# Attention, a dense MLP and a soft mixture of experts on one core: two units opened side by side, a tail with halved copies and staggered loads

## What is computed

```python
for c in range(768 // 32):                    # chunked attention, 4 batches x 8 heads, head size 64
    k_full = concat(mem_k, k[16 before : 32 + 8 after])      # 8 memory keys + up to 56 keys
    a = softmax(q_c @ k_full.T / 8);  out[c] = a @ v_full
x = out as (3072, 512)
h = x @ w_in                                  # 512 x 2048
y = (h * sigmoid(h)) @ w_out                  # 2048 x 512
logits = y @ phi                              # 32 slots
slot_in = softmax(logits over tokens).T @ y   # (32, 512)
slot_out[e] = relu(slot_in[e] @ w1[e]) @ w2[e]       # 8 experts, 4 slots each, 512x1024 and 1024x512
result = softmax(logits over slots) @ slot_out
```

## Time and profile before

| | |
|---|---|
| three runs | 460.40, 461.74, 462.73 us (median 461.74) |
| the profiled execution | 461.4 us |
| its span, first to last instruction | 459.4 us |
| PE busy, share of the span | 442.7 us, 96% |
| PEld / DVE / ACT / POOL busy | 72% / 59% / 30% / 10% |
| mean granted PE clock | 0.994 of full |
| DMA | 81.57 MB, mean 178 GB/s |

### The profile page before, as it was taken

How to read it: one execution, slowest core, us unless ns; L and a number is a source line. 1 busy time by engine, 2 the same in 40 slices (tenths; PEclk the granted TensorE clock), 3 DMA queues, 4 the chain that set the end, 5 groups by cost and what they waited for, 6 DMA issues and landing times.

```text
span 459.4 us, 12251 instructions
## 1 busy us (share of the span) xinstructions
PE 442.7 (96%) x5438; PEld 330.8 (72%) x5438; DVE 272.7 (59%) x528; ACT 138.7 (30%) x257; POOL 47.4 (10%) x44
## 2 busy tenths in 40 slices
PE   6899999999999999999999999999999999999982
PEld 5798877778876778768787777887678779543551
DVE  5677746948477656487584785655664548541133
ACT  2666343232431423223234314233122222210022
POOL 2775100101001001010010010010000000010000
PEclk9999999999999999999999999999999999999997
DMA  8998244023050050230321402226200589999988
GB/s 303 412 414 337 99 156 173 1 93 116 2 201 9 17 191 1 93 118 0 111 97 60 150 1 86 100 93 277 92 0 0 208 358 419 340 418 424 420 357 356
DMA packets 14819, 81.57 MB, mean 178 GB/s; under 512 B 1584, under 2 KB 1712, under 8 KB 8880
## 3 DMA queue, kind: packets, MB, share of 16 engines
q1 hardware_dynamic: 14768, 80.81, 45.5%
HBM read 74.51 MB, written 6.29 MB: 176 GB/s over the span
## 4 chain that ended last, share of the span: by engine, by line
PE 89%; DMA 8%; DVE 1%; issue 0%; ACT 0%; DVEq 0%
PE h_ps L327 59%; DMA unit<-w 5%; PE lpu_ps L344 4%; PE sx_ps L284 4%; PE lpu_ps L375 4%; PE o_ps L311 3%; DMA qk_sb<-qk 3%; PE pt_ps L297 2%; PE sx_ps L375 2%; PE pt_ps L311 2%; PE h_ps L1081 2%; PE o_ps L1061 1%; PE lpu_ps L385 1%; PE sx_ps L1018 1%; PE h_ps L1018 1%; PE o_ps L344 1%
## 5 line engine op out<-in xcount | busy, mean ns | idle before, releaser
L327 PE MATMUL h_ps<-x_odd,w_pair 128*128 128x512 f32 x576 | 137.6, 395 | 0.0
L601 DVE SCALAR_TENSOR_TENSOR gT<-gT,h_ps 128x512 f32<-128x512 f32 (+1 forms) x112 | 67.8, 605 | 108.4 <-ACT gT L462 108.0
L327 PEld LDWEIGHTS h_ps<-x_odd,w_pair 128*128 128x128 f32 x576 | 106.4, 188 | 29.4 <-issue 5.9
L462 ACT ACTIVATE gT<-h_ps 128x512 f32<-128x512 f32 (+1 forms) x112 | 60.1, 536 | 214.2 <-PE h_ps L327 211.8
L327 PE MATMUL h_ps<-x_even,w_pair 128*128 128x512 f32 x384 | 92.4, 395 | 0.0
L327 PEld LDWEIGHTS h_ps<-x_even,w_pair 128*128 128x128 f32 x384 | 70.7, 188 | 19.6 <-issue 5.0
L609 DVE STREAM_TRANSPOSE gB<-gT 128x512 f32<-128x512 f32 x80 | 54.1, 696 | 0.8
L327 PE MATMUL h_ps<-x_short,w_pair 128*128 128x256 f32 x384 | 50.8, 287 | 0.4 <-DVE x_short L591 0.3
L585 POOL TENSOR_TENSOR sc<-sc,row_stats 128x512 f32<-128x512 f32 (+1 forms) x24 | 24.9, 1036 | 254.0 <-DVE row_stats L579 254.0
L327 PEld LDWEIGHTS h_ps<-x_short,w_pair 128*128 128x128 f32 x384 | 47.3, 191 | 4.6 <-issue 2.3
L472 ACT COPY pt<-pt_ps 64x512 f32<-64x512 f32 x46 | 26.5, 577 | 0.8
(11 more groups left out here) (183 smaller groups left out, 401.4 us busy)
## 6 DMA issues: line engine op xcount, KB each, us to landing
unit<-w SPq DMA_DIRECT2D x29, 1024.0 KB, 9.1
qk_sb<-qk SPq DMA_DIRECT2D x24, 640.0 KB, 5.9
v_sb<-v SPq DMA_DIRECT2D x24, 512.0 KB, 4.8
out<-unit SPq DMA_DIRECT2D x6, 1024.0 KB, 5.7
w_stage<-w_in SPq DMA_DIRECT2D x4, 1024.0 KB, 10.7
unit<-w_outT SPq DMA_DIRECT2D x4, 1024.0 KB, 13.5
unit<-w_out SPq DMA_DIRECT2D x4, 1024.0 KB, 6.0
unit_gT<-w SPq DMA_DIRECT2D x2, 1024.0 KB, 13.7
```

The source lines that it names most:

```text
L327: last = nc.tensor.matmul(h_ps[k % 2][:, 0:TOKS[b]], w_pair[:, k // 2, w, kc, k % 2 * 128:k % 2 * 128 + 128], x[:, lo, kc, 0:TOKS[b]], sta ...
L462: nc.scalar.activation(gt_of(b, k), h_ps[k % 2][:, 0:TOKS[b]], ACT.Tanh, scale=0.5).then_inc(tanh_done, 1)
L601: nc.vector.scalar_tensor_tensor(out=gt_of(b, k), in0=gt_of(b, k), scalar=1.0, in1=h_ps[k % 2][:, 0:TOKS[b]], op0=ALU.add, op1=ALU.mult).t ...
```

## The change

It touches the first 30 us and the last 60. In the first block's opening, unit 1 follows unit 0 step by step instead of one step behind: scores, sums, transposes and values of both come side by side, with own PSUM banks for unit 1 (`tr_of`, `o_of`). DVE normalises units 1 and 2 entirely, POOL all others. w_in(0) is issued ahead of v(0). Low parts 0 and 1 are computed in two halves with a semaphore count each, and low part 0 waits for DVE's normalise(1). Scores(3) and values(2) stand behind chunk 3 instead of chunk 2, and w_hi(2) and w_hi(3) come before tanh of chunks 1 and 2. In the tail, u is folded and copied in two halves of 256 columns (ACT and DVE), the slot inputs are turned and summed by one matmul with the fold matrix, five keep_busy calls are shorter or gone, the loads of the last ten tiles also wait for the tile three before, and the stores begin one tile earlier.

```diff
+STAGGERED = 10
-W_NEXT = {1: 3, 4: 4, 5: 5, 8: 6, 9: 7}
+W_NEXT = {1: 2, 2: 3, 4: 4, 5: 5, 8: 6, 9: 7}
-FIRST_SCORES = {2: 3, 6: 4, 10: 5, 11: 6, 13: 7}
-FIRST_VALUES = {2: 2, 6: 3, 10: 4, 13: 5}
+FIRST_SCORES = {3: 3, 6: 4, 10: 5, 11: 6, 13: 7}
+FIRST_VALUES = {3: 2, 6: 3, 10: 4, 13: 5}
...
         def pe_probs_T(pe, u):
-            pe.wait_ge(p_done, u + 1)
-            if u == 1:
-                pe.wait_ge(p_half, 1)
-            if u:
-                pe.wait_ge(pt_done, 2 * u)
+            if u in (1, 2):
+                pe.wait_ge(p_dve, u)
+            else:
+                pe.wait_ge(p_done, u - 1 if u else 1)
+            if u >= 2:
+                pe.wait_ge(pt_done, halves(u))
+                pe.wait_ge(pt_second, 2)
...
-            if b == 0 and q % 2 == 0:
-                pe.wait_ge(wl_done, 2 * n + q // 2 + 1)
+            if b == 0 and (k < 4 or q % 2 == 0):
+                pe.wait_ge(wl_done, k + 1 if k < 4 else k // 2 + 3)
...
         def low_part(ops, eng, m, done):
             eng.wait_ge(wh_done, m + 1)
-            ops.tensor_tensor(w_pair[:, m, 1, :, :], stage[:, m, 1, :, :], w_pair[:, m, 0, :, :].bitcast(fp32),
-                              ALU.subtract).then_inc(done, 1)
+            if m == 0:
+                eng.wait_ge(p_dve, 1)
+            for cols in (slice(0, 128), slice(128, 256)) if m < 2 else (slice(0, 256),):
+                ops.tensor_tensor(w_pair[:, m, 1, :, cols], stage[:, m, 1, :, cols], w_pair[:, m, 0, :, cols].bitcast(fp32),
+                                  ALU.subtract).then_inc(done, 1)
...
                 dve_g(dve, 0, k)
+                if k == 0:
+                    dve_sums(dve, 2)
+                    normalise(nc.vector, dve, 2, p_dve)
...
             load_qk(1)
-            load_v(0)
             sp.wait_ge(qk_in[0], 16)
             load_w_in(0)
+            load_v(0)
...
                 sp.wait_ge(s, count)
+                if u >= NU - STAGGERED:
+                    sp.wait_ge(unit_in[u - 3], 16)
                 sp.dma_start(units[where][:], sources[u]).then_inc(unit_in[u], 16)
...
-            sp.wait_ge(unit_in[NU - 2], 16)
+            sp.wait_ge(unit_in[NU - 3], 16)
...
-                normalise(nc.gpsimd, pool, n, 0, 4 if n == 1 else 2 * PAIRS, p_done)
+                if n not in (1, 2):
+                    normalise(nc.gpsimd, pool, n, p_done)
...
             act_exp(act, 1)
+            act_wh(act, 0)
             act_pt(act, 0)
-            act_wh(act, 0)
+            act_pt(act, 1)
             act_x(act, 0)
+            act_x(act, 1)
             act_wh(act, 1)
-            act_pt(act, 1)
-            act_x(act, 1)
             act_exp(act, 2)
-            act_wh(act, 2)
...
             dve_first_scores(dve)
+            dve_scores(dve, 1)
             dve_sums(dve, 0)
-            dve_scores(dve, 1)
-            pt_half(dve, nc.vector.tensor_copy, 0, 1)
             dve_sums(dve, 1)
-            normalise(nc.vector, dve, 1, 4, 2 * PAIRS, p_half)
+            normalise(nc.vector, dve, 1, p_dve)
+            pt_half(dve, nc.vector.tensor_copy, 0, 1, pt_second)
+            pt_half(dve, nc.vector.tensor_copy, 1, 1, pt_second)
             dve_x(dve, 0)
-            pt_half(dve, nc.vector.tensor_copy, 1, 1)
+            dve_x(dve, 1)
             dve_scores(dve, 2)
-            dve_x(dve, 1)
-            dve_sums(dve, 2)
...
             pe_scores(pe, 0)
-            keep_busy(2, h_ps[0])
             pe_scores(pe, 1)
             keep_busy(8, h_ps[0])
             pe_probs_T(pe, 0)
-            keep_busy(4, h_ps[0])
+            pe_probs_T(pe, 1)
             pe_values(pe, 0)
-            pe_probs_T(pe, 1)
+            pe_values(pe, 1)
             pe_scores(pe, 2)
-            pe_values(pe, 1)
-            keep_busy(4, h_ps[0])
+            keep_busy(1, h_ps[0])
...
-            nc.scalar.copy(uf[:], pt_ps[:]).then_inc(uf_cp, 1)
+            nc.scalar.copy(uf[:, 0:256], uf_ps[0][:, 0:256]).then_inc(uf_act, 1)
             act.wait_ge(uT_tr, 1)
-            nc.scalar.copy(uT, s_ps[:]).then_inc(uT_done, 1)
+            nc.scalar.copy(uT[:, 0:256], uT_ps[0][:, 0:256]).then_inc(uT_act, 1)
...
             for kc in range(KC):
-                last = nc.tensor.transpose(s_ps[:, kc * 128:(kc + 1) * 128], si_part[:, kc * 128:(kc + 1) * 128], ident[:])
+                last = nc.tensor.matmul(s_ps[:, kc * SLOTS:(kc + 1) * SLOTS], si_part[:, kc * 128:(kc + 1) * 128],
+                                        fold[:, 0:SLOTS], start=True, stop=True)
```

More of the change, by code:

```diff
@@ L225, in moe_program @@
         last_u_act, last_u_dve, foldd_done = sem("last_u_act"), sem("last_u_dve"), sem("foldd_done")
-        uf_mm, uf_cp, uT_tr, uT_done, si_mm, si_cp, si_tr, siT_done = (
-            sem(x) for x in ("uf_mm", "uf_cp", "uT_tr", "uT_done", "si_mm", "si_cp", "si_tr", "siT_done"))
+        uf_mm, uf_act, uf_dve, uT_tr, uT_act, uT_dve, si_mm, si_cp, si_tr, siT_done = (
+            sem(x) for x in ("uf_mm", "uf_act", "uf_dve", "uT_tr", "uT_act", "uT_dve", "si_mm", "si_cp", "si_tr", "siT_done"))
         ffn1_mm, relu_act, relu_dve, hid_tr, hT_done, hT_zero, ffn2_mm, so_cp, so_mm, so_done = (
@@ L263, in o_of, with tr_of, halves @@
         def o_of(u):
+            if u == 1:
+                return lu_ps
             return pt_ps if u >= PAIRED and u % 2 else o_ps
+        def tr_of(u):
+            return lp_ps if u == 1 else pt_ps
+        def halves(n):
+            return n if n <= 2 else 2 * n - 2
         def heads(ap):
@@ L296, in pe_probs_T @@
             for j in range(4):
-                last = nc.tensor.transpose(pt_ps[:, j * 128:(j + 1) * 128],
+                last = nc.tensor.transpose(tr_of(u)[:, j * 128:(j + 1) * 128],
                                            sc_u(u)[:, 2 * j:2 * j + 2, :].rearrange("p c k -> p (c k)"), ident[:])
@@ L462, in act_tanh, with pt_half @@
             nc.scalar.activation(gt_of(b, k), h_ps[k % 2][:, 0:TOKS[b]], ACT.Tanh, scale=0.5).then_inc(tanh_done, 1)
-        def pt_half(eng, copy, u, c):
+        def pt_half(eng, copy, u, c, done):
             eng.wait_ge(p_tr, u + 1)
@@ L472, in pt_half @@
             copy(pt_u(u)[half, :, c * CHUNK:(c + 1) * CHUNK],
-                 pt_ps[half, :].rearrange("p (j q) -> p j q", q=CHUNK)).then_inc(pt_done, 1)
+                 tr_of(u)[half, :].rearrange("p (j q) -> p j q", q=CHUNK)).then_inc(done, 1)
         def act_pt(act, u):
-            pt_half(act, nc.scalar.copy, u, 0)
+            pt_half(act, nc.scalar.copy, u, 0, pt_done)
             if u >= UNITS[0]:
-                pt_half(act, nc.scalar.copy, u, 1)
+                pt_half(act, nc.scalar.copy, u, 1, pt_done)
         def act_exp(act, u):
@@ L579, in dve_sums, with normalise @@
             nc.vector.reciprocal(rinv[:, i, :], rsum[:, i, :]).then_inc(rinv_done, 1)
-        def normalise(ops, eng, u, lo, hi, done):
+        def normalise(ops, eng, u, done):
             eng.wait_ge(rinv_done, u + 1)
-            p = sc_u(u)[:, lo:hi, :]
-            ops.tensor_tensor(p, p, rinv[:, u % SB, lo:hi].unsqueeze(2).to_broadcast([128, hi - lo, WIN]),
+            ops.tensor_tensor(sc_u(u), sc_u(u), rinv[:, u % SB, :].unsqueeze(2).to_broadcast([128, 2 * PAIRS, WIN]),
                               ALU.mult).then_inc(done, 1)
@@ L1043, in _ @@
             pe.wait_ge(raw_kept, 4 * NB)
-            for i in range(4):
-                nc.tensor.matmul(pt_ps[32 * i:32 * i + 32, :], foldd, acc[:, i, :], start=True, stop=False)
+            for half in range(2):
+                for i in range(4):
+                    nc.tensor.matmul(uf_ps[half][32 * i:32 * i + 32, 0:256], foldd, acc[:, i, 256 * half:256 * half + 256],
+                                     start=True, stop=False)
             pe.wait_ge(last_u_act, 2)
             pe.wait_ge(last_u_dve, 2)
-            for i in range(4):
-                last = nc.tensor.matmul(pt_ps[32 * i:32 * i + 32, :], fold[:, 0:SLOTS], last_u[:, i, :], start=False, stop=True)
+            for half in range(2):
+                for i in range(4):
+                    last = nc.tensor.matmul(uf_ps[half][32 * i:32 * i + 32, 0:256], fold[:, 0:SLOTS],
+                                            last_u[:, i, 256 * half:256 * half + 256], start=False, stop=True)
             last.then_inc(uf_mm, 1)
-            keep_busy(3, h_ps[0])
-            pe.wait_ge(uf_cp, 1)
+            keep_busy(2, h_ps[0])
             for g in range(4):
-                last = nc.tensor.transpose(s_ps[:, g * 128:(g + 1) * 128], uf[:, g * 128:(g + 1) * 128], ident[:])
+                pe.wait_ge((uf_act, uf_dve)[g // 2], 1)
+                last = nc.tensor.transpose(uT_ps[g // 2][:, g % 2 * 128:g % 2 * 128 + 128], uf[:, g * 128:(g + 1) * 128], ident[:])
             last.then_inc(uT_tr, 1)
-            keep_busy(3, h_ps[0])
-            pe.wait_ge(uT_done, 1)
+            keep_busy(2, h_ps[0])
             for g in range(NF):
+                pe.wait_ge((uT_act, uT_dve)[g // 2], 1)
                 tile = wait_unit(pe, g)
```

20 lines of the change are left out of this document (13 added, 7 removed).

## The result

The changed kernel takes 466.63 us (median of five runs, 465.34 to 469.04) where the kernel before takes 461.17 on the same chip (five runs, 460.4 to 462.73): 1.0114 times as long, 95% interval 1.0087 to 1.0141. By the ratio it is slower by 5.3 us. I had forecast 462.5 within 459.4 to 464.8 and given "slower" 0.19. The profiled execution of it took 465.63, with a span of 463.4 and a mean granted clock of 0.985 (before: 461.4, 459.4, 0.994).

A forecast was written before the change was run, and what follows sets the result against it. Bound by the MLP, 59% of the span, with the start's loads and last weight tile's DMA at its ends; 461.4 + 1.3 (start, block included) + 0 (fold, stagger) - 0.2 (stores) = 462.5 us, range 459.4 to 464.8.

The forecast's parts named there:

- X: Opening: moment when DVE begins scores(2), taken as 16.8 us, the middle of 16.5 to 17.1.
- The loads: Opening: with w_in(0) ahead of v(0), loads come 0.4 to 0.8 us late.
- The block of normalise(2): First chunks: DVE's normalise(2) waits for the end of POOL's low(2), 1.7 us; forecast case 462.5, chance 0.35.
- The course without a block: First chunks, rival: normalise(2) not held by POOL, chunk 6 ends at X + 15.3; 460.8 us, chance 0.28.
- blocked twice: First chunks, rival: sums(2)'s tensor_scalar stands too, then low(3) precedes normalise(2); 2.6 us more, 465.1, chance 0.10.
- T: First chunks: start of tanh(0) on ACT, put at X + 2.2 us.
- The clock: Before the first chunk, rival: longer PE gaps lower the clock, costing 2 to 3 us; 464.5 to 465.5, chance 0.07.
- The shift goes unchanged to the end: After chunk 6: the opening's shift passes unchanged to 399.36 us and through the DMA stream to the end.
- Halves and turn: Tail: PE reaches ffn1 0.5 to 0.9 us earlier, but the DMA stream covers it, worth 0.
- Stagger: Tail: the last ten loads' added waits never run the slowest DMA engine dry; worth 0, bounds -0.3 to +0.5 us.
- early stores: Tail: three stores start 2.4 us earlier in the DMA hole, the fourth gains at most 0.3; taken as -0.2.
- The late engines: Last tile, rival: half the slowest DMA engines' 3 us lag goes; 459.3 without block, 461.0 with; chance 0.20.

The follow-up runs named there:

- no_epsilon: The changed kernel without the tensor_scalar that adds 1e-9 to unit 2's row sums; 466.07 us, ratio 1.0080 to the kernel before.
- pool_waits: The changed kernel with GpSimd waiting for VectorE's normalise(2) before low part 2; 461.18 us, ratio 0.9956 to the kernel before.
- clock_held_16: The changed kernel without staggered loads, plus sixteen idle matmuls ahead of unit 2's transposes; 464.44 us, ratio 1.0067 to the kernel before.
- fold_alone: The kernel before with only the halves of u, the fold as turn and fewer idle matmuls; 461.15 us, ratio 0.9992.
- tail_only: The kernel before with the changed tail, staggered loads included; 463.37 us, ratio 1.0004.
- stagger_alone: The kernel before with only the waits of the last ten loads on the tile three before; 461.96 us, ratio 1.0005.

## Why the prediction was wrong, step by step

- **X and the start of the first chunk: right.** 16.52 and 16.62, within the 16.5 to 17.1 given and 0.3 earlier than my middle. The loads are the term that was off: I had them 0.4 to 0.8 late, and w_in(1) landed at 18.1 (issued 7.19, 10.9 to landing; before 18.24, forecast 18.9) and v(1) at 13.94 (before 14.10, forecast 14.7), so nothing was late. "Side by side" does what it says, and 2.5 us are won there. A first sign of what follows is in this stretch too: the tensor_scalar of unit 1 at 10.64 took 0.64 beside GpSimd's multiplication.
- **The block of normalise(2): right in kind and size, and priced once.** no_epsilon shows my forecast's own course: the multiplication held to the end of low(2), chunk 6 at X + 16.5 (33.05 with X = 16.51) for X + 17.0. The course without a block was X + 14.8 in pool_waits (31.54 with X = 16.71) for X + 15.3. The half microsecond lies ahead of chunk 3 in both: the stall of 0.7 that I had there without a block isn't in pool_waits, where chunk 3 starts at X + 5.4 for X + 5.9.
- **The failed step: the tensor_scalar ahead of it was counted at its unheld time, 0.17.** It took 2.33. I had it as the rival "blocked twice", with 2.34 + 0.3 and a chance of 0.10, and set against it that GpSimd "needs a moment between two instructions". Its own condition was "if POOL starts before T + 1.6"; my times said T + 1.4 for low(2) and T + 1.6 for the tensor_scalar, so by my own sum the condition held, by 0.2. In the trace it held by 0.07. What was left was whether such an operation is held at all, and for that I had no row; the chance should have been near that of the forecast. The Trainium skill had it: SBUF — State Buffer, section "Who interferes with whom", names `tensor_scalar` among the operations that can take the shared ports, where their operands meet its conditions for a two-port mode, and says that tensor_reduce never contends on this chip. The 2.33 at 19.96 agrees with the first. With the second agrees that GpSimd's multiplication at 10.21 took its 1.04 as everywhere, though a tensor_reduce of scores in SBUF ran beside it until 10.60. I had used the rule for two inputs only.
- **The clock: the mechanism right, the place wrong.** I had it fall before the first chunk, by shorter gaps; it stayed at 1.00 there. It fell after the block, in a wait of 3.99, and cost 1.2 (clock_held_16) to 1.6 (the changed kernel against pool_waits). I had not put the two slow rivals together: 465.1 + 1.2 to 1.6 is 466.3 to 466.7. Each rival had its chance alone, though one makes the other. That the median of 466.63 lies there is partly luck: the sum is one for the profiled execution, which took 465.63, and errors cancel in it. At chunk 6 it gives +3.9 for both held instructions; X was 0.3 earlier, the path to chunk 3 0.5 shorter, the second hold 2.3 for 2.6, and the clock added 1.6, which makes the 4.5 measured to 0.1.
- **The wait for probs_T(3): right.** 0.85 forecast; 0.84 at 34.97 in the changed kernel.
- **"The shift goes unchanged to the end": nearly.** 4.48 at chunk 6, 4.4 at the 21st tile, 3.6 at the last tile, where the slowest DMA engine was less behind. (The stream starts with the 21st tile at 398.98; my sum began it at 399.36, the 22nd.)
- **Halves and turn worth 0, covered by the DMA: right.** fold_alone 0.9992. Their size without the cover was overrated: TensorE reaches ffn1 at 409.20 in tail_only against 409.46, 0.26 instead of 0.5 to 0.9.
- **Stagger 0 (-0.3 to +0.5), early stores -0.2: right on the kernel before, not in general.** stagger_alone 1.0005. That "most engines [...] just keep running" is false: the first engine loses 0.2 to 3 us against every trace without the stagger. Mostly the slowest engine sets the end and hides it; in no_epsilon the one long wait cost another 1.6 by the clock. The early stores brought nothing that a run shows, and no run has them alone. The fourth store, which I had gaining up to 0.3, took 4.45 in the changed kernel against 3.97.
- **The late engines: half of the lag went, and the time didn't follow.** The changed kernel's slowest engine was 1.8 behind and not 3.6, as the rival had it; a change of this lag was my own sign of being wrong. The first engine, 0.9 slower, took half of it back. The size is the trace's own: it spreads from 1.7 to 4.2 over fourteen traces.

What stays open: what makes one DMA engine fall back by 1.5 us (I had named the instruction fetches; no run takes them away), and why the fourth store's slowest engine is 0.3 behind in one trace and 2.5 in another. Together they are larger than what the tail's edits could bring.

## What to carry to other kernels

When a change puts VectorE's work beside GpSimd's, go through every VectorE instruction of the pair, the small ones too, and ask who begins first: a held 128x8 instruction cost as much here as a held 128x512 one, and the next one can be held again by GpSimd's next. If the order can be fixed by a wait on the engine that has slack, fix it (here 1.5 us of GpSimd's slack bought 5.45 at chunk 6). Rivals that cause one another (a block, then an idle TensorE, then its clock) must be added in one case, not listed apart.
